# First product: the low-weight pass over features 128 to 191 on 64 rows, two d_ff tiles on the array's two row halves

## The reference, cut to what matters

```python
# x: 4 x 4096 x 192, weight_gen: 4 x 4096 x 8 heads x 7 taps
w = exp(weight_gen - max over taps); w = w / (sum over taps + 1e-9)
a[b, s, h, g] = sum over k of w[b, s, h, k] * x_padded[b, s + k, h, g]   # x with 6 rows of zeros ahead
a = a.reshape(16384, 192)
h = a @ w_in                     # 192 x 2048
g = s * relu(h) ** 2 + b
out = g @ w_out                  # 2048 x 192
```

## Time and profile before

| What | Value |
|---|---|
| Median of three runs | 1239.95 us (1239.42 to 1240.96) |
| Span of the profiled execution, first to last instruction | 1238.8 us |
| PE matmul busy | 1208.1 us, 98% |
| PE weight loads busy | 1098.3 us, 89% |
| VectorE busy | 966.5 us, 78% |
| ScalarE busy | 757.7 us, 61% |
| GpSimd busy | 187.3 us, 15% |
| Mean granted TensorE clock | 0.992 of full speed |

### The profile page before, as it was taken

The page is one execution under the profiler, slowest core; times in us unless marked ns, Lnnn a source line. Parts: engine busy times, 40 slices in busy tenths (PEclk is TensorE's granted clock), DMA queues, the critical chain, the costliest instruction groups (busy, mean ns, idle before and its releaser), DMA issues.

```text
span 1238.8 us, 18906 instructions
## 1 busy us (share of the span) xinstructions
PE 1208.1 (98%) x6880; PEld 1098.3 (89%) x6880; DVE 966.5 (78%) x1130; ACT 757.7 (61%) x812; POOL 187.3 (15%) x97
## 2 busy tenths in 40 slices
PE   3799999999999999999999999999999999999998
PEld 3699998999998999999999999999999999999998
DVE  6887778887778887778787778877778877778843
ACT  3456656656665666665665665665666665566564
POOL 7411011110011110111110111110111110111110
PEclk8899999999999999999999999999999999999999
DMA  6111101111101111101111101111101111001000
GB/s 190 36 49 35 49 16 45 48 48 35 48 13 48 48 48 35 48 13 48 48 43 41 48 13 48 48 35 48 40 21 48 48 35 48 27 34 48 13 1 26
DMA packets 17892, 51.51 MB, mean 42 GB/s; under 512 B 2140, under 2 KB 8539, under 8 KB 17882
## 3 DMA queue, kind: packets, MB, share of 16 engines
q1 hardware_dynamic: 17733, 50.80, 11.9%
q10 hardware_dynamic: 149, 0.59, 0.2%
HBM read 38.79 MB, written 12.58 MB: 41 GB/s over the span
## 4 chain that ended last, share of the span: by engine, by line
PE 96%; DVE 2%; POOL 1%; DMA 0%; issue 0%; ACTq 0%; ACT 0%; DVEq 0%; POOLq 0%
PE hp L627 47%; PE op L640 33%; PE op L642 15%; PE hp L611 1%; PE hp L614 1%; DMA x_in<-in_x 0%; POOL tap_pool L312 0%; POOL acc L321 0%; DVE x_in L187 0%; DVE g_lo L527 0%; DVE acc L498 0%; DVE acc L483 0%; DVE tap L483 0%; DVE out_sb L544 0%; DVE w_exp L451 0%
## 5 line engine op out<-in xcount | busy, mean ns | idle before, releaser
L640 PE MATMUL op<-wo,g_hi 128*128 128x384 f32 x2048 | 598.4, 362 | 7.0 <-DVE g_lo L527 7.0
L627 PE MATMUL hp<-xT,w_hi 128*128 128x512 f32 x1536 | 522.9, 395 | 1.9 <-DVE xT L511 1.9
L642 PE MATMUL op<-wo,g_lo 128*128 128x192 f32 x2048 | 514.2, 251 | 0.0
L378 ACT ACTIVATE r<-hp 128x1024 f32<-128x1024 f32 x256 | 260.4, 1017 | 360.0 <-PE hp L627 351.4
L527 DVE TENSOR_TENSOR g_lo<-r,g_hi 128x1024 fp32r<-128x1024 f32 x256 | 343.5, 1342 | 98.0 <-ACT g_hi L389 93.5
L627 PE MATMUL hp<-xT,w_lo 128*128 128x512 f32 x1024 | 402.8, 393 | 0.0
L642 PEld LDWEIGHTS op<-wo,g_lo 128*128 128x128 f32 x2048 | 393.2, 192 | 4.5
L640 PEld LDWEIGHTS op<-wo,g_hi 128*128 128x128 f32 x2048 | 385.9, 188 | 11.0 <-issue 7.4
L627 PEld LDWEIGHTS hp<-xT,w_hi 128*128 128x128 f32 x1536 | 279.5, 189 | 56.0 <-DVE xT L511 2.3
L382 ACT ACTIVATE r<-r 128x1024 f32<-128x1024 f32 x256 | 271.2, 1059 | 7.1
L627 PEld LDWEIGHTS hp<-xT,w_lo 128*128 128x128 f32 x1024 | 192.9, 188 | 42.9
(11 more groups left out here) (40 smaller groups left out, 270.8 us busy)
## 6 DMA issues: line engine op xcount, KB each, us to landing
x_in<-in_x SPq DMA_DIRECT2D x30, 960.0 KB, 4.8
out<-out_sb SPq DMA_DIRECT2D x31, 384.0 KB, 2.3
w_in<-in_weight_gen SPq DMA_DIRECT2D x32, 112.0 KB, 2.0
wo_raw<-in_moe_w_out SPq DMA_DIRECT2D x4, 384.0 KB, 7.9
w_raw<-in_moe_w_in SPq DMA_DIRECT2D x4, 256.0 KB, 6.4
w_raw<-in_moe_w_in SPq DMA_DIRECT2D x8, 128.0 KB, 6.3
x_in<-in_x SPq DMA_DIRECT2D x1, 768.0 KB, 8.1
x_in<-in_x ACTq DMA_DIRECT2D x1, 540.0 KB
```

Of the source, the lines that this page charges most:

```text
L378: nc.scalar.activation(r[:, b, :], hp[:, PAIR * b:PAIR * (b + 1), :], ACT.Relu).then_inc(relu_done, 1)
L627: mm = nc.tensor.matmul(hp[:, j, :], w[:, f], xt, start=(n == 0), stop=(n == len(passes) - 1))
L640: nc.tensor.matmul(op[:, t, 0:2 * D], g_hi[:, g % 2, j, cols], wo[:, k, :, :].rearrange("p a d -> p (a d)"), start=(k == 0), stop=False)
L642: mm = nc.tensor.matmul(op[:, t, 0:D], g_lo[:, g % 2, j, cols], wo[:, k, 0, :], start=False, stop=(k == FT - 1))
```

## The change

- A new tile `xT2_up` holds in its rows 64 to 127 a copy of the high part of x of features 128 to 191. ScalarE makes it as the last part of `hi_of_attn`, after a wait for its own copies, and raises `t_up_ready`.
- The w2_lo pass now multiplies the low weights by the high part of x only, with 64 rows. Tile j of a pair takes array rows 0 to 63 (weights and xT2 from partitions 0 to 63), tile j + 1 rows 64 to 127 (weights and xT2_up from partitions 64 to 127). The product of low weight and low x is no longer in the sum.
- The order in `first_product` is another: the four full passes of all four tiles first, then the four 64-row matmuls in the order j = 0, 1, 2, 3; `h_ready` is raised after the second and the fourth of them. In group 0 TensorE waits for `t_up_ready` ahead of them.

```diff
+        xT2_up = sb("xT2_up", [P, N], F32R)
...
                 high.then_inc(t_hi_ready, 1)
+                act.wait_ge(t_hi_ready, 2 * i + 2)
+                nc.scalar.activation(xT2_up[D2:P, :], xT2[0:D2, :].bitcast(F32), ACT.Copy).then_inc(t_up_ready, 1)
...
             def first_product(i, g, first=False):
+                cols = [slice((g * GROUP + j) * P, (g * GROUP + j + 1) * P) for j in range(GROUP)]
                 for j in range(GROUP):
                     q = 2 * g + j // PAIR
                     if j % PAIR == 0 and not (first and q < 2):
                         pe.wait_ge(relu_done, i * PAIRS + q - 1)
-                    f = slice((g * GROUP + j) * P, (g * GROUP + j + 1) * P)
-                    passes = [(w1_hi, xT1[:, 0, :]), (w1_hi, xT1[:, 1, :]), (w1_lo, xT1[:, 0, :]),
-                              (w2_hi, xT2[:, :]), (w2_lo, xT2[:, :])]
+                    passes = [(w1_hi, xT1[:, 0, :]), (w1_hi, xT1[:, 1, :]), (w1_lo, xT1[:, 0, :]), (w2_hi, xT2[:, :])]
                     for n, (w, xt) in enumerate(passes):
-                        mm = nc.tensor.matmul(hp[:, j, :], w[:, f], xt, start=(n == 0), stop=(n == len(passes) - 1))
-                    if j % PAIR == PAIR - 1:
-                        mm.then_inc(h_ready, 1)
+                        nc.tensor.matmul(hp[:, j, :], w[:, cols[j]], xt, start=(n == 0), stop=False)
+
+                if g == 0:
+                    pe.wait_ge(t_up_ready, i + 1)
+                for j in range(0, GROUP, PAIR):
+                    nc.tensor.matmul(hp[:, j, :], w2_lo[0:D2, cols[j]], xT2[0:D2, :], start=False, stop=True)
+                    nc.tensor.matmul(hp[:, j + 1, :], w2_lo[D2:P, cols[j + 1]], xT2_up[D2:P, :], start=False,
+                                     stop=True).then_inc(h_ready, 1)
```

More of the change, by code:

```diff
@@ L149, in mix_and_mlp @@
         t_lo_ready = sem("t_lo_ready")
+        t_up_ready = sem("t_up_ready")
         h_ready = sem("h_ready")
```

## The result

The changed kernel takes 1265.7 us (median of 4 runs, 1265.6 to 1266.9) against 1240.1 (4 runs, 1239.4 to 1241.0): ratio 1.0208, 95% interval 1.0196 to 1.0221. The direction was forecast, and 1265.7 lies in the range; the forecast of 1251.5 was too low: it had +11.4 us where +25.6 was measured.

A forecast was written before the change was run, and what follows sets the result against it. TensorE's own stream was taken as the bound, with little slack. Saved matmul slots, shape changes and the later announcement made +0.38 us in 30 steps, plus 0.75, less 0.72: +11.4, about 1251.5 us; range 1229 to 1282.

The forecast's parts named there:

- What bounds the kernel, and where the wait would arise: TensorE's own stream bounds the kernel; after the change it waits 1.25 us before the transposes of each step.
- e + q: Cost on TensorE of entering (e) and leaving (q) 64-row work in each group, taken as 0.14 us each.
- Two slots saved by full overlap: In each group's w2_lo pass, four TensorE slots become two: 0.46 us per group, 1.84 per step.
- The announcement: h_ready of a group's even pair moves to the seventeenth slot, so its relu starts 1.60 us later.
- Sg: Start time of the first product of group g in a step; S2 is 613.72 in the kernel before.
- rival 2: Full drain and uncovered load at each change of array shape, 0.30 us each: 1282 us; chance 0.20.
- the formula: Step time of the changed kernel: 37.05 + 3e + 2q, giving 37.75 us at 0.14 each.
- The slack of 0.2 us before the next step: At the next step's head, xT's low parts are ready at S2 + 19.56, TensorE comes at 19.75: wait hidden.
- The copy at no cost: ScalarE's added copy xT2_up, priced 0.6 us, is hidden; without cover 0.6 us a step, 19 us in all.
- rival 4: TensorE's clock falls in the new wait, costing 2.5 us per step: 1327 us; chance 0.02.
- Rival 3: The halves of a pair don't overlap on TensorE: 1267 us with free shape changes, 1297 otherwise; chance 0.10.
- The break-even: The whole kernel becomes faster than before if 3e + 2q is below 0.32.

The follow-up runs named there:

- The order alone: Kernel before with only the new order: all matmuls full, the four w2_lo ones after the sixteen others, no xT2_up; 1271.3 us, ratio 1.0250.
- the same-half run: Changed kernel with both tiles of a pair on array rows 0 to 63, xT2_up made but not read; 1316.8 us, ratio 1.0618.

## Why the prediction was wrong in size

- *What bounds the kernel, and where the wait would arise*: right. The wait stands ahead of the transposes in all 31 steps that have them, and its two releasers are level, as the forecast's sums make them for e + q near 0.43: attn_b ends at 640.39 + 0.42 = 640.81, relu 6 at 639.76 + 1.02 = 640.78.

```profile
639.76 1.02 ACT L382 ACTIVATE r<-hp 128x1024 f32<-128x1024 f32 x1 [3.83 <-PE hp L636]
```
```profile
640.39 0.42 DVE L507 TENSOR_TENSOR attn_b<-acc,tap 128x256 f32<-128x256 f32 x1
```

  The order alone makes this wait, and the two runs that announce h early have none. Forecast were 1.25 us of waiting, counted from the end of a slot; counted so it is 640.94 - (639.55 + 0.23) = 1.16, and the profile's 0.99 counts from the end of the last record.
- *Two slots saved by full overlap*: right (starts 0.01 us apart; the same-half run lacks it).
- *The announcement*: Sg + 4.12 + e was forecast. With the measured e of 0.20 that is 4.32; 630.63 - 626.30 = 4.33 was measured, 1.81 us later than before and not 1.60 (the 1.60 left e out):

```profile
630.63 1.03 ACT L382 ACTIVATE r<-hp 128x1024 f32<-128x1024 f32 x1 [3.91 <-PE hp L636]
```

- **The mis-sized term is the price of the shape changes**: "I take 0.14 each, the uncovered weight load alone". Measured are 0.20 and 0.21. The load itself shows 0.11 in the spacing, less than the 0.14 of the transposes' load in the earlier trace rows; what I left out is the 0.09 to 0.10 before it, in which nothing loads. The sign that the prediction names for e and q, the spacing of starts less 0.23, shows just this part (630.09 - 629.77 and 630.75 - 630.42: 0.09 and 0.10) and misses the load behind it; the price is read from the next start. The truth lay between my value and rival 2's 0.30, which had a full tail of 0.16 and a full load of 0.14. In the formula the step goes from 37.75 to 37.05 + 3 x 0.20 + 2 x 0.21 = 38.07. That is 0.32 of the 0.46 us per step that are missing (38.21 - 37.75): 0.06 us of error counts five times in each of 31 steps.
- **A term was missing**: the return from a wait. From the transposes to the next step are 5.26 instead of 5.21 us and group 0 is 9.18 instead of 9.13, by the reading above each time a load that nothing covers; and the transposes start at S2 + 14.64 (640.94 - 626.30), where the forecast's 14.40 + e gives 14.60. Together 0.14 us per step, the rest. The run with the order alone has as much without any half-array matmul (0.17 per step).
- *The slack of 0.2 us before the next step*: with e and q as measured, xT's low part ends 0.86 behind 645.20, at 646.06, and the step begins at 646.20. No idle time of the matmuls shows there, but the step's first weight load starts only 0.02 us ahead of its matmul, and in the kernel before 0.08 ahead (632.64 to 632.72):

```profile
646.18 0.30 PEld L630 LDWEIGHTS hp<-xT,w_hi 128*128 128x128 f32 x2
```
```profile
632.64 0.30 PEld L627 LDWEIGHTS hp<-xT,w_hi 128*128 128x128 f32 x2
```

  So "hidden" was not quite right, and this is the 0.05 us of group 0 above. The run with later transposes shows this wait as the next one behind the first.
- *The copy at no cost*: right, shown alone. *The clock*: 1.00 through the new gap; rival 4 is out. Rival 3 is out by the starts.
- *The break-even*: 3e + 2q is 1.02 here and would have had to be below about 0.35 by the forecast's sum, below about 0.2 with the missing 0.14.
- *The number*: 1265.7 is also within 2 us of rival 3's 1267, in which the halves don't overlap at all. The time alone could not have told the two apart; the starts in a pair and the run on the same half do.

The Trainium skill's sentence that changing the tiling mode drains TensorE (TensorEngine Tiling (Array Packing), Key Properties) agrees in kind with this trace: the changes looked at show 0.09 to 0.10 us without a load or a new matmul, and between the two tiles of a pair there are 0.01 us. Its price by the rows is 0.20 us with the load, less than the tail and load records added up. How much of the 0.09 us is the emptying of the array and how much is issue was not taken apart; the ends of matmuls are modelled, and no run varied it.

## What to carry to other kernels

Before asking what a shorter instruction saves, ask when the last instruction of its group signals: a signal 1.8 us later cost 31 us here, while the packed matmuls, less their shape changes, are worth 0.05 to 0.08 us per group, 6 to 10 us in all. If a cheap phase must be separate from the rest, try it at the head of the accumulation, not at its end: the same matmuls went from 26 us slower to 10 us faster. And when a signal moves, follow every wait behind it: with the first wait gone, the second took its place at the same cost. Count changes of array shape as items with a price (0.2 us each here), and pack enough half-array work between them to pay for two; two pairs of 512 columns only just do (0.46 saved, 0.38 to 0.41 paid).

## What the runs showed of the hardware that was not expected

- Two 64-row matmuls on different row halves start 0.01 us apart and take one slot of 0.23 us together; on the same half each takes 0.23 us, like a 128-row one.
- A change between 128-row and 64-row work costs about 0.20 us in either direction (0.38 to 0.41 for both): 0.09 to 0.10 us until the next weight load begins, then some 0.11 us of load in the open. Within a shape the loads are hidden again from the second on.
- A wait costs TensorE more than its length: the first record behind it is 0.05 to 0.08 us longer than its like (0.65 against 0.60 for the transposes, 0.71 and 0.72 against 0.64 at the head of a step). That this is the weight load in the open is a reading of the rows; no run varied it.
